# Norms of the expert embeddings made during the attention and spread through memory, with the logits scaled early

## The reference

```python
xn = x / (np.linalg.norm(x, axis=-1, keepdims=True) + 1e-06)
en = expert_emb / (np.linalg.norm(expert_emb, axis=-1, keepdims=True) + 1e-06)
logits = xn @ en.T / tau
expert_idx = np.argmax(logits, axis=1)
...
gate_w = probs[np.arange(N), expert_idx]
```

## Time and profile before

| | us |
|---|---|
| median of 3 runs (lowest, highest) | 829.52 (828.16, 829.99) |
| profiled execution | 828.33 |
| its span | 826.6 |
| PE, DVE, ACT, POOL busy | 805.7, 362.8, 323.6, 140.1 |

### The profile page before, as it was taken

How to read it: one execution, slowest core, us unless ns; L and a number is a source line. 1 busy time by engine, 2 the same in 40 slices (tenths; PEclk the granted TensorE clock), 3 DMA queues, 4 the chain that set the end, 5 groups by cost and what they waited for, 6 DMA issues and landing times.

```text
span 826.6 us, 14410 instructions
## 1 busy us (share of the span) xinstructions
PE 805.7 (97%) x5348; PEld 731.4 (88%) x5349; DVE 362.8 (44%) x590; ACT 323.6 (39%) x616; POOL 140.1 (17%) x206
## 2 busy tenths in 40 slices
PE   5999998799999999999999999999999999999998
PEld 4999987799999999997888888888888888888887
DVE  6788887855544545355532322232222223222221
ACT  5677766544534445455522322222222212212211
POOL 4444440414232413000000100010010001001001
PEclk9999999799999999999999999999999999999999
DMA  9877762565562555220000100010010001000001
GB/s 204 194 207 199 193 189 71 126 218 203 199 206 88 189 195 184 84 77 2 1 1 1 39 0 1 1 39 0 1 39 1 1 0 39 1 1 15 24 1 39
DMA packets 32574, 67.60 MB, mean 82 GB/s; under 512 B 12145, under 2 KB 21390, under 8 KB 31374
## 3 DMA queue, kind: packets, MB, share of 16 engines
q1 hardware_dynamic: 28174, 55.93, 22.5%
q0 software_dynamic: 4352, 11.04, 4.2%
HBM read 57.48 MB, written 9.48 MB: 81 GB/s over the span
## 4 chain that ended last, share of the span: by engine, by line
PE 96%; DVE 1%; DMA 1%; issue 1%; ACT 0%; POOL 0%; DVEq 0%
PE low_banks L1056 18%; PE scores L1056 18%; PE sums L1063 9%; PE high_banks L1063 9%; PE sums L998 9%; PE low_banks L987 6%; PE scores L987 6%; PE high_banks L998 4%; PE scores L823 3%; PE sums L839 3%; PE high_banks L812 2%; PE low_banks L798 2%; PE sums L830 2%; PE low_banks L806 1%; PE high_banks L850 1%; PE low_banks L967 1%
## 5 line engine op out<-in xcount | busy, mean ns | idle before, releaser
L574 POOL DMA_INDIRECT out<-out_sb,placed x24 | 23.3, 970 | 470.5 <-ACT out_sb L769 464.7
L1056 PE MATMUL low_banks<-x_hi,wab_hi 128*128 128x512 f32 x216 | 84.1, 389 | 1.0 <-issue 1.0
L1056 PE MATMUL low_banks<-x_hi,wab_lo 128*128 128x512 f32 x216 | 84.7, 392 | 0.0
L1056 PE MATMUL scores<-x_hi,wab_lo 128*128 128x512 f32 x216 | 84.7, 392 | 0.0
L1056 PE MATMUL scores<-yT_lo,wab_hi 128*128 128x512 f32 x216 | 84.6, 392 | 0.0
L1056 PE MATMUL low_banks<-yT_lo,wab_hi 128*128 128x512 f32 x216 | 84.6, 392 | 0.0
L1056 PE MATMUL scores<-x_hi,wab_hi 128*128 128x512 f32 x216 | 84.0, 389 | 0.0
L1450 DVE TENSOR_TENSOR h<-low_banks,a_sb 128x512 f32<-128x512 f32 x36 | 24.9, 692 | 133.9 <-ACT a_sb L752 133.9
L1450 DVE TENSOR_TENSOR h<-scores,a_sb 128x512 f32<-128x512 f32 x36 | 24.9, 692 | 130.4 <-ACT a_sb L752 118.0
L752 ACT ACTIVATE a_sb<-low_banks 128x512 f32<-128x512 f32 x36 | 21.5, 597 | 139.3 <-PE low_banks L1056 139.3
L752 ACT ACTIVATE a_sb<-scores 128x512 f32<-128x512 f32 x36 | 21.5, 597 | 134.7 <-PE scores L1056 134.7
(11 more groups left out here) (233 smaller groups left out, 1856.3 us busy)
## 6 DMA issues: line engine op xcount, KB each, us to landing
w_raw<-in_w SPq DMA_DIRECT2D x8, 1536.0 KB
w_raw<-in_w SPq DMA_DIRECT2D x32, 384.0 KB
tok<-in_tok SPq DMA_DIRECT2D x48, 192.0 KB, 3.2
qk_all<-in_chan SPq DMA_DIRECT2D x48, 192.0 KB, 3.4
xd<-xst SPq DMA_DIRECT2D x24, 192.0 KB, 1.9
wab_raw<-in_wab SPq DMA_DIRECT2D x6, 768.0 KB, 6.6
wout_raw<-in_wout SPq DMA_DIRECT2D x1, 1536.0 KB, 6.7
wout_raw<-in_wout SPq DMA_DIRECT2D x1, 768.0 KB, 4.3
```

Source lines behind the costliest of these rows:

```text
L574: pool.indirect_dma_start(out=out, out_offset=bass.IndirectOffsetOnAxis(ap=placed[:, u * B + t, 0:1].bitcast(i32), axis=0), in_=out_sb[:, ...
L1056: last_op = pe.matmul(bank[2 * i + m][:, :], w[:, KM * m + k, cols], moving, start=(k == 0 and w is wab_hi and x is not None), stop=(k == ...
```

## The change

1. In chunk 0 DVE's sum of squares starts from 1e-30 in place of 0.
2. After chunk 0 ACT makes exp(0.5 ln s) and exp(-0.5 ln s) of the 8 sums s (`Ln`, `Exp`, `Exp`, each 8x1). POOL makes a root of them with one step of Newton's method and adds the 1e-6 (two instructions, 8x1).
3. SP stores the 8 norms to a table in memory before the last loaded chunk, and in that chunk loads them back to all 128 partitions.
4. In the drain DVE inverts them after the logits of tile 20 and multiplies the logits of tiles 0 to 20 by them, in place. `EARLY` is now 21.
5. POOL multiplies the 8 embedding columns of `back` by the inverse norms once tile 20's logits are made, and PE waits for that before tile 21. So the logits of the last three tiles come scaled out of PE.
6. The root, the diagonal, the PE product and the copy out of PSUM are gone, and so is the multiply in `best_first`.
7. `best_first` and `best_second` of the first 21 tiles stand ahead of DVE's branch. Before, those of the first 20 stood behind it, between the logits of the last three tiles.

```diff
-    EARLY = TILES - B
+    EARLY = TILES - B + 1
...
+    norm_table = nc.dram_tensor("norm_table", [E], fp32, kind="Internal").ap()
...
+                if tail and b == 2:
+                    sp_eng.wait_ge(norms_stored, 16)
+                    sp_eng.dma_start(r["norm8"][:, :], norm_table.rearrange("(a e) -> a e", a=1).to_broadcast([P, E])).then_inc(norms_loaded, 16)
...
+        sp_eng.wait_ge(emb_steps, 2)
+        sp_eng.dma_start(norm_table.rearrange("(e o) -> e o", o=1), r["embn"][0:E, 5:6]).then_inc(norms_stored, 16)
         chunk(C - 1, tail=True)
...
+        def refine_norms():
+            root = r["embn"]
+            pool.wait_ge(emb_rooted, 2)
+            pool.tensor_scalar(root[0:E, 4:5], root[0:E, 0:1], root[0:E, 3:4], root[0:E, 2:3], ALU.mult, ALU.add).then_inc(emb_steps, 1)
+            pool.wait_ge(emb_steps, 1)
+            pool.tensor_scalar(root[0:E, 5:6], root[0:E, 4:5], 0.5, 1e-6, ALU.mult, ALU.add).then_inc(emb_steps, 1)
...
         chunk(C, last=True)
+        pool.wait_ge(norms_inverted, 1)
+        pool.wait_ge(xz_done, TILES - B + 1)
+        pool.tensor_tensor(back[:, :, 2 * D:], back[:, :, 2 * D:], r["inv8"][:, :].rearrange("p (a e) -> p a e", a=1).to_broadcast([P, HP, E]),
+                           ALU.mult).then_inc(back_scaled, 1)
...
                     if last and b == 0:
-                        act.wait_ge(emb_squared, 1)
-                        act.activation(r["embn"][0:E, 1:2], r["embn"][0:E, 0:1], ACT.Sqrt).then_inc(emb_norm, 1)
-                        act.wait_ge(emb_norm, 1)
-                        act.activation(r["diag"][0:E, :], ident[0:E, 0:E], ACT.Copy, scale=r["embn"][0:E, 1:2], bias=1e-6 / E).then_inc(norms_ready, 1)
...
-                                act.wait_ge(norms_spread, 1)
-                                act.activation(r["norm8"][:, :], bank[7][:, 448:448 + E], ACT.Copy).then_inc(norms_kept, 1)
...
         chunk(0, first=True)
+        act.wait_ge(emb_squared, 1)
+        act.activation(r["embn"][0:E, 1:2], r["embn"][0:E, 0:1], ACT.Ln).then_inc(emb_norm, 1)
+        act.wait_ge(emb_norm, 1)
+        act.activation(r["embn"][0:E, 2:3], r["embn"][0:E, 1:2], ACT.Exp, scale=0.5).then_inc(emb_rooted, 1)
+        act.activation(r["embn"][0:E, 3:4], r["embn"][0:E, 1:2], ACT.Exp, scale=-0.5).then_inc(emb_rooted, 1)
...
-            pe.wait_ge(norms_ready, 1)
             pe.wait_ge(x_ready, TILES - 2)
-            pe.matmul(bank[7][:, 448:448 + E], ones[0:E, :], r["diag"][0:E, :], start=True, stop=True).then_inc(norms_spread, 1)
...
+            pe.wait_ge(back_scaled, 1)
             rows_and_logits(TILES - 3, 1, last_xz[1])
...
             logits(TILES - 4, xz)
+            dve.wait_ge(norms_loaded, 16)
+            dve.reciprocal(r["inv8"][:, :], r["norm8"][:, :]).then_inc(norms_inverted, 1)
+            dve.wait_ge(norms_inverted, 1)
+            dve.wait_ge(z_kept, EARLY)
+            unscaled = r["z"][:, 0:EARLY, :]
+            link(dve.tensor_tensor(unscaled, unscaled, over(row(r["inv8"][:, :]), [P, EARLY, E]), ALU.mult))
             mask(TILES - 2, 2)
...
+            best_first(0, EARLY, link)
+            best_second(0, EARLY, link)
 
         def finish_tiles():
...
             logits(TILES - 3, last_xz[1])
             logits(TILES - 2, last_xz[2])
-            best_second(0, EARLY, link)
             logits(TILES - 1, last_xz[3])
```

More of the change, by code:

```diff
@@ L179, in attention_moe_ffn @@
                             first=[P, TILES, E], r=[P, TILES], oh=[P, E, TILES],
-                            z=[P, TILES, E], zn=[P, TILES, E], v=[P, E, TILES], v2=[P, E, TILES],
+                            z=[P, TILES, E], v=[P, E, TILES], v2=[P, E, TILES],
                             slotf=[P, TILES], cum=[P, E + 1], many=[P, E, SIZES], nt=[P, E], nt1=[P, E],
@@ L192, in attention_moe_ffn @@
     kT = [sb(f"kT{b}", [P, HP, P]) for b in range(B)]
-    for name, shape in dict(emb2=[P, HP * P], embn=[P, 4], emb3=[P, HP, 2, 64], diag=[P, E], norm8=[P, E], inv8=[P, E]).items():
+    for name, shape in dict(emb2=[P, HP * P], embn=[P, 6], emb3=[P, HP, 2, 64], norm8=[P, E], inv8=[P, E]).items():
         r[name] = sb("r_" + name, shape)
@@ L236, in attention_moe_ffn @@
     embT_done = sem("embT_done")
-    emb_squared, emb_ready, norms_ready, norms_spread, norms_kept = map(
-        sem, ("emb_squared", "emb_ready", "norms_ready", "norms_spread", "norms_kept"))
+    emb_squared, emb_rooted, emb_steps, emb_ready, norms_stored, norms_loaded, norms_inverted, back_scaled = map(
+        sem, ("emb_squared", "emb_rooted", "emb_steps", "emb_ready", "norms_stored", "norms_loaded", "norms_inverted", "back_scaled"))
     zero_written = sem("zero_written")
@@ L527, in _ @@
         later_constants()
+        refine_norms()
         with pool.Fori(1, C) as c:
@@ L635, in chunk @@
                             act.activation(yt[m % 2][:, :, :, :].rearrange("p i j t -> p i (j t)"), of[:, :, 0:2 * P], ACT.Copy).then_inc(y_kept, 1)
-                            if m == TILES - 2:
-                                act.wait_ge(norms_spread, 1)
-                                act.activation(r["norm8"][:, :], bank[7][:, 448:448 + E], ACT.Copy).then_inc(norms_kept, 1)
         chunk(0, first=True)
+        act.wait_ge(emb_squared, 1)
[3 more added lines that the diff above has]
+        act.activation(r["embn"][0:E, 3:4], r["embn"][0:E, 1:2], ACT.Exp, scale=-0.5).then_inc(emb_rooted, 1)
         with act.Fori(1, C) as c:
@@ L904, in last_chunk @@
             pe.wait_ge(steep_ready, 1)
+            pe.wait_ge(back_scaled, 1)
             rows_and_logits(TILES - 3, 1, last_xz[1])
-            pe.wait_ge(norms_kept, 1)
             rows_and_logits(TILES - 2, 2, last_xz[2])
@@ L1112, in square_embeddings @@
             flat = r["emb3"][0:E, :, :, :].rearrange("p a h d -> p (a h d)")
-            dve.tensor_tensor_reduce(r["emb2"][0:E, :], flat, flat, 1.0, 0.0, ALU.mult, ALU.add, r["embn"][0:E, 0:1]).then_inc(emb_squared, 1)
+            dve.tensor_tensor_reduce(r["emb2"][0:E, :], flat, flat, 1.0, 1e-30, ALU.mult, ALU.add, r["embn"][0:E, 0:1]).then_inc(emb_squared, 1)
         dve.wait_ge(const_ready, FOR_DVE)
@@ L1128, in best_first @@
             three = [P, high - low, E]
-            products = r["zn"][:, some, :]
-            then(dve.tensor_tensor(products, r["z"][:, some, :], over(row(r["inv8"][:, :]), three), ALU.mult))
+            products = r["z"][:, some, :]
             then(dve.tensor_reduce(r["m"][:, some], products, AX.X, ALU.max))
@@ L1219, in last_chunk @@
             dve.tensor_scalar(steep[:, :], bank[6][:, 511:512], P - 0.5, None, ALU.is_lt).then_inc(steep_ready, 1)
+            dve.wait_ge(const_ready, SETUP)
+            best_first(0, EARLY, link)
+            best_second(0, EARLY, link)
         def finish_tiles():
-            dve.wait_ge(const_ready, SETUP)
-            dve.wait_ge(z_kept, EARLY)
-            dve.wait_ge(norms_kept, 1)
-            link(dve.reciprocal(r["inv8"][:, :], r["norm8"][:, :]))
-            best_first(0, EARLY, link)
             logits(TILES - 3, last_xz[1])
             logits(TILES - 2, last_xz[2])
-            best_second(0, EARLY, link)
             logits(TILES - 1, last_xz[3])
```

## The result

| | before | after |
|---|---|---|
| median of 21 runs each (lowest, highest), us | 829.27 (827.46, 830.06) | 830.43 (827.89, 831.57) |
| ratio, 95% interval | | 1.0017 (1.0010, 1.0024) |
| profiled execution, us | 828.33 | 830.32 |
| its span, mean granted clock of PE | 826.6, 0.993 | 829.0, 0.989 |

What follows compares the result with a forecast made beforehand. PE holds 96% of the chain, so gains lie only where it is held up, in drain and sort. Profiled 828.33 us less 0.2 is 828.1, against the median 829.3; range 827.9 to 831.0.

Steps and rivals of the forecast that it cites:

- Front, memory, POOL: New steps after chunk 0, the norms' store and load, and POOL's scaling of `back`: taken to cost 0.
- PE's product removed: In the drain, the norms' PE product leaves the chain: 0.31 us, tile 21 starting at 130.76 in place of 131.07.
- DVE's side 0.93 us earlier: In the sort, DVE's 17 pieces of `in_low` end at 142.80 in place of 143.73.
- ACT becomes late, PE gains 0.2 and not 0.93: ACT waits for tile 21 behind DVE's branch, 0.37 us later; its `in_low` comes last, the sort ending at 143.96.
- over 0.5 us earlier: Sign against the forecast: the sort's last product on PE ends more than 0.5 us earlier.
- The whole gain: Rival, 12%: ACT's hole shrinks or ends with something fixed, DVE sets the sort, gain 0.93 us, 828.6.
- a slow DVE branch: Rival, 9%: DVE's hole at its branch is 2.73 us in place of 1.72, sort ends 0.8 later, 830.3.
- late norms: Rival, 3%: the norms' load sits behind expert weights over 6.5 us, stopping DVE and PE; 2 us gives 831.5.
- From there to the end everything moves along, the gather, the transposes and the PE-bound remainder: Step behind the sort: all that follows moves with PE's gain of 0.2 us.
- Clock or another shift late 6%: Rival, 6%: the clock or another shift makes the kernel slower, counted as over 1.7 us.
- the 9% for slower: Chance of being slower by more than 1.7 us: 6% late clock or shift plus 3% late norms; with scatter 10%.
- an early one: Rival, 6%: the clock or another shift comes early, counted as faster by more than 1.7 us.

Runs made afterwards that it cites:

- d_dve19: Changed kernel with 19 in place of 17 columns of `in_low` on DVE and 5 in place of 7 on ACT: 829.83 us, ratio 1.0009.
- a_order: Changed kernel with the one-hot of 21 tiles put back behind DVE's branch, norms still through memory: 828.58 us, ratio 0.9989.
- b_fill10: Kernel before with 10 in place of 3 products that keep PE going ahead of the first gather: 828.89 us, ratio 0.9993.
- f_best: Changed kernel with w2 loads held until the ninth `in_low` column, 19 columns on DVE, 10 PE-filling products ahead of the gather: 827.84 us, ratio 0.9990.
- c_w2_late: Changed kernel with SP's loads of w2 held until the ninth column of `in_low` in place of the first: 828.90 us, ratio 0.9999.
- d_dve19_w2: Changed kernel with 19 columns of `in_low` on DVE and the w2 loads held until the sixth column: 829.13 us, ratio 0.9989.
- e_dve19_w2_9: Changed kernel with 19 columns of `in_low` on DVE and the w2 loads held until the ninth column: 828.33 us, ratio 0.9991.
- c_after_again: The changed kernel with no edit, run again beside the kernel before: 830.62 us, ratio 1.0017.
- c_warm: Changed kernel with PE-filling products in all three holes between the token transpose and the first expert product: 829.84 us, ratio 1.0009.
- c_order_warm: Changed kernel with the one-hot back behind DVE's branch and more PE-filling products ahead of the gather and behind the third tile: 829.61 us, ratio 1.0004.
- d_w2_first: Changed kernel with the wait for `low_ready` taken out, so the w2 loads are not tied to `in_low`: 829.85 us, ratio 1.0002.

## Why the prediction was wrong, point by point

- **Front, memory, POOL: right.** The two `Exp` and `Ln` took 0.20 us each in ACT's idle time, the norms landed 3.1 us after an issue at 116.82, and the mask still waited 0.49 us for PE. POOL had scaled `back` at 126.3, PE needed it at 130.4.
- **PE's product removed: right.** Tile 21's product starts at 130.41 in place of 131.07. 0.31 of that is the product. The other 0.35 us were there by 24 us already and belong to no step: PE's first product started 0.13 us earlier (4.47, 4.60), and near 23 us four transposes took 0.78 us where they had taken 1.01. The granted clock was 1.00 there in both executions, so it was not the clock; what it was is not shown.
- **DVE's side 0.93 us earlier: right in size.** `in_low` starts 1.34 us earlier; less the 0.35 that is 0.99.
- **ACT becomes late, PE gains 0.2 and not 0.93: right.** The sort's end went from 144.18 to 143.62, 0.56, less 0.35 is 0.21. d_dve19 confirms that ACT was the bound there. By its own sign ("over 0.5 us earlier") the prediction would call itself wrong at 0.56, but that takes the 0.35 in.
- **The whole gain, a slow DVE branch, late norms: none came.** DVE's hole was 1.64 us (in a_order, too, where nothing but the branch is in it), and the norms landed 3.1 us after their issue.
- **"From there to the end everything moves along, the gather, the transposes and the PE-bound remainder": this step failed.** Ahead of the gather stand SP's loads of w2, which the prediction did not name. They are released by the first of DVE's 17 columns, so they take DVE's 0.93 us (SP's shorter way let them), while the gather takes ACT's 0.2. The distance between the two grew from 3.99 to 5.01 us, and with it came the hole ahead of the third tile. The first gather to the first product took 9.53 us in place of 9.05, and the low clock lasted 5.2 us into the products, where it had ended ahead of them. Closing the distance with one number took the loss away (1.0017 to 0.9999); opening it in a_order brought the hole and the low clock back.
- **"Clock or another shift late 6%": this came.** That such a shift costs over 1.7 us, as the 9% for slower has it, no row or run of before shows, nor what an early one would gain. What the runs showed: the clock stood at 0.50 until 159.6 in place of 153.4, 6.2 us longer, and the two profiles differ by 2.4 us in span, the medians by less (1.2), since the kernel before has such runs too; with the clock back at 149.3 (b_fill10) and 148.8 (f_best) the ratios were 0.9993 and 0.9990. Of PE's idle times the long one got shorter (3.93 to 2.55 us), but two new ones came behind it, 0.57 and 1.54 us, where one of 0.79 had been, and they are the ones right ahead of the expert products.
- **The size.** Low-clock runs went from 54 of 153 (35%) to 31 of 33 (94%). In the kernel before, low runs took about 830.0 and those at 0.993 or 0.994 about 828.4. 0.59 of 1.6 us is 0.9 us. Among low runs alone, the changed kernel stood at 830.5 and 830.7, 0.5 to 0.7 above the kernel before (0.4 by the means). Its profile gives 0.3 of that: 0.5 us more from the first gather to the first product, less the 0.2 that the sort gained. Together that is 1.2 to 1.6, where 0.0017 is 1.4; it is an estimate from runs of several sets, and no run measures the two parts one by one.
- The profile before had been taken at 0.993, one side of the kernel's own mixture. The forecast took its low stretch, which ended at 153.4, as if it were a property of the kernel.

Shown: the one-hot's place makes the loss, and most of it goes through the loads of w2, since holding them alone takes the ratio to 0.9999. Loads far ahead bring the hole, the longer way to the first product and, in most runs, the low clock. The rest, between c_w2_late and a_order or d_dve19_w2 (0.9989), fits ACT's late end of the sort, but its size is within the noise. Argued and not shown is that the holes keep the clock low: they went together over all versions, but the profiles of c_w2_late and e_dve19_w2_9 have 17.1 us at a granted clock of 0.50 without the hole, and a_order's has 13.7.

The traces also show how the loads change the gathers. Where the loads were held (c_w2_late), the first gather landed 4.8 us after its issue and the third 3.1. In the changed kernel run beside it (c_after_again) the first landed 3.5 after and the third 5.1; in c_warm it was 3.6 and 4.3. In a_order the third took 3.1 again. So loads far ahead let the first tile in sooner and the third later, and PE's hole is made of both. With the loads 4.5 us or more ahead, PE took the first tile 3.4 to 4.0 us after its gather's issue and the third 3.8 to 5.2 after; with less, the first 4.3 to 5.5 after, and the third without a wait but in c_order_warm. Open is why: what passes between the loads and the gathers in the queues. Open, too, is what makes the first product late. In all eight kernels that waited for the third tile it stood 2.95 to 3.00 us behind that tile's start, and 2.09 to 2.21 us where there was no wait (at 0.50). The rows of `x_lo` say that its data were there (0.97 us ahead of it in the kernel after), and no run shows what fills that time.

## What to carry to other kernels

When a step moves, list every DMA whose release hangs on it, also those far from the critical path, and ask how their distance to the next transfer on the path changes. A stretch in which PE waits just ahead of a long dense part can be worth more than its own length, since the clock at which the dense part starts went with it here (0.50 until 159.6 in place of 153.4). The sum of the holes does not tell it: from the sort to the first product PE stood idle for 4.7 us in the kernel after (2.55, 0.57, 1.54) and 4.8 in c_w2_late (4.13, 0.70), and the low runs were 31 of 33 and 5 of 12. And where runs of one kernel show two levels of mean clock, one profile shows one of them: look at the share of each before taking a duration from it.

## What had not been expected of the hardware

- The same program comes with mean clocks of 0.989 to 0.994, 1.6 us apart in time. What differs in the profiles is how long PE stays at a granted clock of 0.50 around the gather, until 153.4 before and 159.6 after, and in the profile of c_w2_late, which had no hole ahead of the third tile, until 158.8.
- SP's way from its last store through the branch and the waits for its stores to the next DMA took 5.8 us before and 3.8 us after (d_w2_first), though its own instructions there are nearly the same. ACT's hole at its branch was 2.73 and 2.84 us, DVE's 1.64 (a_order; before 1.72 with the norms' wait).
- Four gathers behind 1.5 MB of loads don't land at even distances: first and third took 4.8 and 3.1 us with the loads held, 3.5 and 5.1 with the loads 1.3 us further ahead.
- If PE has to wait for the third tile, the first product comes 2.99 us behind that tile's start; if PE still has earlier tiles to work on, 2.10 (with the tiles at a granted clock of 0.50; in three profiles with them at 1.00 it is 2.64 to 2.87). What the 0.9 us between the two are made of, no run shows.
